# Attention and two feed-forward layers: q and k of a head loaded once, split in one tile, and copied on chip

## The reference

```python
B, H, S, D = 2, 8, 768, 64                      # 16 heads
q_bucket = sum((q @ proj > 0) * 2 ** arange(6)) # 6 hash bits for each row of q, and k_bucket of k
scores = q @ k.T / 8, or -1e9 where q_bucket != k_bucket
attn = exp(scores - max) / (sum + 1e-9)
x = (attn @ v) as 1536 tokens x 512
h = x @ w_in; g = 0 below -1, h above 1, (h + 1) ** 2 / 4 between; x = g @ w_out   # 512 -> 2048 -> 512
h = x @ w2_in; g = h - tanh(h); out = g @ w2_out
```

## Time and profile before

| | us |
|---|---|
| median of 3 runs | 813.68 (813.03 to 814.91) |
| span of the profiled execution, first to last instruction | 810.5 |
| what lies around the span, by the median | 3.2 |
| TensorE busy | 772.8 |
| attention, about | 0 to 273 |

### The profile page before, as it was taken

How to read it: one execution, slowest core, us unless ns; L and a number is a source line. 1 busy time by engine, 2 the same in 40 slices (tenths; PEclk the granted TensorE clock), 3 DMA queues, 4 the chain that set the end, 5 groups by cost and what they waited for, 6 DMA issues and landing times.

```text
span 810.5 us, 11750 instructions
## 1 busy us (share of the span) xinstructions
PE 772.8 (95%) x3712; PEld 636.0 (78%) x3712; DVE 417.4 (51%) x757; ACT 358.6 (44%) x701; POOL 326.5 (40%) x267
## 2 busy tenths in 40 slices
PE   4899999999998999999999999999999999999997
PEld 2688788788787888878887888878888888888885
DVE  2889888888898466343334455551222221231222
ACT  2788788788796343333323323331122221221221
POOL 4779789789798997000000066680000000000000
PEclk8999999999999999999999999999999999999999
DMA  6523423433221333000000022320000100010001
GB/s 202 174 89 103 147 83 103 128 102 103 78 79 53 123 114 128 1 1 0 1 1 0 0 78 104 103 79 1 0 1 1 52 0 0 0 52 0 0 0 52
DMA packets 17864, 47.25 MB, mean 58 GB/s; under 512 B 2288, under 2 KB 4464, under 8 KB 17840
## 3 DMA queue, kind: packets, MB, share of 16 engines
q1 hardware_dynamic: 17840, 46.94, 18.0%
HBM read 38.87 MB, written 3.15 MB: 52 GB/s over the span
## 4 chain that ended last, share of the span: by engine, by line
PE 71%; DVE 10%; issue 7%; POOL 4%; ACT 4%; DMA 1%; DVEq 1%; SPq 0%; ACTq 0%; POOLq 0%
PE ps L489 33%; PE ps L564 29%; PE ps L466 4%; DVE p_lo L743 3%; DVE clamped L727 2%; PE ps L423 2%; POOL probs L346 2%; POOL k_b L331 2%; PE ps L480 1%; ACT probs L610 1%; ACT p_hi L620 1%; DVE x_pair L754 1%; DVE g_raw L805 1%; DVE row_den L735 1%; DMA k_raw<-kk 1%
## 5 line engine op out<-in xcount | busy, mean ns | idle before, releaser
L489 PE MATMUL ps<-x_hi,w 128*128 (+1 forms) x768 | 255.0, 396 | 0.0
L813 DVE TENSOR_TENSOR g_lo<-g_raw,g_hi 128x512 fp32r<-128x512 f32 x96 | 71.0, 739 | 269.4 <-ACT g_hi L692 269.4
L692 ACT ACTIVATE g_hi<-g_raw 128x512 fp32r<-128x512 f32 x96 | 60.8, 633 | 296.2 <-PE ps L564 267.3
L489 PEld LDWEIGHTS ps<-x_hi,w 128*128 128x128 f32 x768 | 144.4, 188 | 33.9
L489 PE MATMUL ps<-x_lo,w 128*128 (+1 forms) x384 | 152.1, 396 | 0.0
L564 PE MATMUL ps<-g_hi,w 128*128 128x512 f32 x384 | 125.6, 391 | 3.4 <-DVE g_lo L813 3.4
L564 PE MATMUL ps<-w,g_hi 128*128 128x512 f32 x384 | 118.6, 390 | 0.0
L303 POOL TENSOR_SCALAR w<-stage 128x1024 fp32r<-128x1024 f32 x32 | 38.1, 1189 | 166.0 <-PE ps L564 164.5
L743 DVE TENSOR_TENSOR p_lo<-ps,p_hi 128x384 fp32r<-128x384 f32 x192 | 97.8, 550 | 12.6 <-ACT p_hi L620 11.4
L466 PE MATMUL ps<-ident,probs 128*128 128x128 f32 x576 | 86.3, 282 | 16.9 <-DVE p_lo L743 12.6
L346 POOL TENSOR_SCALAR probs<-probs,row_inv 128x768 f32<-128x768 f32 x96 | 86.8, 907 | 38.6 <-DVE row_inv L737 37.5
(11 more groups left out here) (48 smaller groups left out, 896.7 us busy)
## 6 DMA issues: line engine op xcount, KB each, us to landing
stage<-weights SPq DMA_DIRECT2D x32, 512.0 KB, 3.3
qk_raw<-qk SPq DMA_DIRECT2D x16, 384.0 KB, 3.5
q_raw<-qq SPq DMA_DIRECT2D x16, 384.0 KB, 3.1
k_raw<-kk SPq DMA_DIRECT2D x16, 384.0 KB, 3.9
q_a<-q_b SPq DMA_DIRECT2D x16, 192.0 KB
v_raw<-v SPq DMA_DIRECT2D x16, 192.0 KB, 2.5
out<-stage SPq DMA_DIRECT2D x12, 256.0 KB, 2.4
q_b<-bits SPq DMA_DIRECT2D x16, 54.0 KB
```

What stands on the lines that cost most here:

```text
L489: last = nc.tensor.matmul(ps[:, f % H_BANKS, :], w[:, f, wp, k * P:(k + 1) * P], xs[:, :, k, bass.ds(t * TOK, TOK)], start=(k == 0 and wp ...
L692: nc.scalar.activation(g_hi[:, slot, :], g_raw[:, slot, :], ACT.Copy).then_inc(g_hi_ready, 1)
L813: nc.vector.tensor_tensor(g_lo[:, slot, :], g_raw[:, slot, :], g_hi[:, slot, :].bitcast(F32), ALU.subtract).then_inc(g_split, 1)
```

## The change

The loads `qq` and `kk` go, `qk` (q over k, 128 rows) stays. It is scaled (rows of q by -0.125, rows of k by 1) into `qk_scaled`, rounded into `qk_hi` and subtracted into `qk_lo`, each once for q and k together, on GpSimd. Six copies on chip then bring 64 rows each to where the products read them (`copy_hi`: four, `copy_lo`: two). `qk_scaled`, `qk_hi` and `qk_lo` have one buffer, so the rounding of a head waits until the six copies of the head before have landed. The scores wait for the six parts and the two bit copies, the threshold for the bit copies of the odd head. ScalarE no longer rounds k. The hash bits of heads 0 and 1 come from products of their own (`first_products`), the first split is shared by VectorE, ScalarE and GpSimd. All pairs are written out on every engine in place of the loop. The core of the diff:

```diff
-            q_raw = sb("q_raw", [P, 2, S], F32, att)
-            k_raw = sb("k_raw", [P, 2, S], F32, att)
             qk_raw = sb("qk_raw", [P, 2, S], F32, att)
+            qk_scaled = sb("qk_scaled", [P, S], F32, att)
+            qk_hi = sb("qk_hi", [P, S], F32R, att)
+            qk_lo = sb("qk_lo", [P, S], F32R, att)
...
+            bits_odd = sb("bits_odd", [HROWS, S], F32R, att)
...
         @block.sync
         def _(sp):
             def load_qk(h, s):
-                for dst, src in ((q_raw, qq), (k_raw, kk)):
-                    sp.dma_start(dst[:, s, :], src[h, :, :]).then_inc(qk_loaded[s], 16)
+                sp.dma_start(qk_raw[:, s, :], qk[h, :, :]).then_inc(qk_loaded[s], 16)
 
             def load_v(h, s):
                 sp.dma_start(v_raw[:, s, :, :].rearrange("p t d -> p (t d)"), v[h, :, :]).then_inc(v_loaded[s], 16)
 
-            def load_pair(p):
-                for s in range(2):
-                    sp.dma_start(qk_raw[:, s, :], qk[2 * p + s, :, :]).then_inc(pair_loaded, 16)
-
-            def copy_q_hi(s):
-
-                sp.dma_start(q_a[0:D, s, :].bitcast(F32), q_b[0:D, s, :].bitcast(F32)).then_inc(rows_copied[s], 16)
-
-            def copy_bits(s):
+            def copy_hi(eng, s):
+
+                for dst, row, src in ((q_a, 0, 0), (k_a, 0, D), (k_a, D, D), (q_b, 0, 0)):
+                    eng.dma_start(dst[row:row + D, s, :].bitcast(F32), qk_hi[src:src + D, :].bitcast(F32))\
+                        .then_inc(parts_copied[s], 16)
+
+            def copy_lo(s):
+
+                for dst, row, src in ((q_a, D, 0), (k_b, 0, D)):
+                    sp.dma_start(dst[row:row + D, s, :].bitcast(F32), qk_lo[src:src + D, :].bitcast(F32))\
+                        .then_inc(parts_copied[s], 16)
+
+            def copy_bits(s, src):
 
                 for r, dst in enumerate((q_b, k_b)):
-                    row = s * HROWS + r * MROWS
                     sp.dma_start(dst[D:D + MROWS, s, :].bitcast(F32),
-                                 bits[row:row + MROWS, :].bitcast(F32)).then_inc(rows_copied[s], 16)
+                                 src[r * MROWS:(r + 1) * MROWS, :].bitcast(F32)).then_inc(bits_copied[s], 16)
+
+            def bit_rows(s):
+                return bits[s * HROWS:(s + 1) * HROWS, :]
 
             sp.dma_start(mask_s[:, :], mask_consts[:, :]).then_inc(const_loaded, 16)
-            load_pair(0)
             load_qk(0, 0)
             load_qk(1, 1)
+            sp.wait_ge(qk_hi_ready, 1)
+            copy_hi(sp, 0)
             sp.wait_ge(qk_split, 1)
-            copy_q_hi(0)
-            sp.wait_ge(bits_ready, 2)
-            copy_bits(0)
+            copy_lo(0)
+            sp.wait_ge(first_bits, 2)
+            copy_bits(0, bits[0:HROWS, :])
             load_v(0, 0)
             load_v(1, 1)
-            sp.wait_ge(bits_product, 2)
-            load_pair(1)
-            sp.wait_ge(first_k_split, 1)
+            sp.wait_ge(scale_done, 1)
+            sp.wait_ge(first_product, 4)
             load_qk(2, 0)
+            sp.wait_ge(scale_done, 2)
+            load_qk(3, 1)
 
             def pair(p):
+                first = isinstance(p, int) and p == 0
                 last = isinstance(p, int) and p == PAIRS - 1
                 before = isinstance(p, int) and p == PAIRS - 2
                 sp.wait_ge(qk_split, 2 * p + 2)
-                copy_q_hi(1)
-                copy_bits(1)
+                wait_from(sp, scores_ready, PT_TILES * p)
+                copy_hi(sp, 1)
+                copy_lo(1)
+                if first:
+                    sp.wait_ge(first_bits, 4)
+                copy_bits(1, bits_odd[:, :] if first else bit_rows(1))
                 if last:
                     return
-                load_qk(2 * p + 3, 1)
+                sp.wait_ge(qk_split, 2 * p + 3)
+                sp.wait_ge(scores_ready, PT_TILES * p + QT)
+                copy_hi(sp, 0)
+                copy_lo(0)
                 sp.wait_ge(v_split, 2 * p + 1)
                 load_v(2 * p + 2, 0)
-                if not before:
-                    sp.wait_ge(bits_product, 2 * p + 4)
-                    load_pair(p + 2)
-                sp.wait_ge(bits_ready, 2 * p + 4)
-                sp.wait_ge(qk_split, 2 * p + 3)
-                copy_q_hi(0)
-                copy_bits(0)
+                sp.wait_ge(bits_ready, 2 * p + 2)
+                copy_bits(0, bit_rows(0))
                 if not before:
                     load_qk(2 * p + 4, 0)
                 sp.wait_ge(v_split, 2 * p + 2)
                 load_v(2 * p + 3, 1)
-
-            with sp.Fori(0, PAIRS - 2) as p:
+                if not before:
+                    sp.wait_ge(scale_done, 2 * p + 4)
+                    load_qk(2 * p + 5, 1)
+
+            pair(0)
+            for p in range(1, PAIRS):
                 pair(p)
-            pair(PAIRS - 2)
-            pair(PAIRS - 1)
 
             def load_w(c, i):
...
-            def scale_q(p, s):
-
-                wait_alone(pool, qk_loaded[s], 32 * (p + 1), pool_passed)
-                pool.tensor_scalar(q_raw[:, s, :], q_raw[:, s, :], -0.125, 1.0, ALU.mult, ALU.mult)\
-                    .then_inc(q_scaled, 1)
-
-            def low_q(s):
-
-                return pool.tensor_tensor(q_a[:, s, :], q_raw[:, s, :], q_b[:, s, :].bitcast(F32), ALU.subtract)
-
-            def split_q(p, s, tiles_before):
-
-                wait_alone(pool, scores_ready, tiles_before, pool_passed)
-                wait_alone(pool, q_scaled, 2 * p + s + 1, pool_passed)
-                pool_round(q_b[:, s, :], q_raw[:, s, :]).then_inc(q_hi_ready, 1)
-                pool.wait_ge(q_hi_ready, 2 * p + s + 1)
-                low_q(s)
-
-            def split_k(p, s):
-
-                pool.wait_ge(k_hi_ready, 2 * p + s + 1)
-                pool.tensor_tensor(k_b[:, s, :], k_raw[:, s, :], k_a[:, s, :].bitcast(F32), ALU.subtract)\
+            def scale_qk(p, s):
+
+                wait_alone(pool, qk_loaded[s], 16 * (p + 1), pool_passed)
+                wait_alone(pool, qk_split, 2 * p + s, pool_passed)
+                pool.tensor_scalar(qk_scaled[:, :], qk_raw[:, s, :], qk_scale, 1.0, ALU.mult, ALU.mult)\
+                    .then_inc(scale_done, 1)
+
+            def hi_qk(p, s):
+
+                wait_alone(pool, parts_copied[1 - s], 96 * (p + s), pool_passed)
+                pool.wait_ge(scale_done, 2 * p + s + 1)
+                pool_round(qk_hi[:, :], qk_scaled[:, :]).then_inc(qk_hi_ready, 1)
+
+            def lo_qk(p, s):
+
+                pool.wait_ge(qk_hi_ready, 2 * p + s + 1)
+                pool.tensor_tensor(qk_lo[:, :], qk_scaled[:, :], qk_hi[:, :].bitcast(F32), ALU.subtract)\
                     .then_inc(qk_split, 1)
...
                         if n == 0:
-                            split_q(p, 1, PT_TILES * p)
+                            hi_qk(p, 1)
                         if n == 1:
-                            split_k(p, 1)
-                        if n == 3:
+                            lo_qk(p, 1)
+                        if n == 3 and not last:
+                            scale_qk(p + 1, 0)
+                        if n == 4 and not last:
+                            hi_qk(p + 1, 0)
+                        if n == 5 and not last:
+                            lo_qk(p + 1, 0)
+                        if n == 6:
                             split_v(p, 0)
-                        if n == 4 and not last:
-                            scale_q(p + 1, 0)
-                        if n == 6 and not last:
-                            split_q(p + 1, 0, PT_TILES * p + QT)
-                        if n == 7 and not last:
-                            split_k(p + 1, 0)
-                        if n == 10 and not last:
-                            scale_q(p + 1, 1)
-                        if n == 11:
+                        if n == 10:
                             split_v(p, 1)
+                        if n == 11 and not last:
+                            scale_qk(p + 1, 1)
...
-            scale_q(0, 0)
-            pool.wait_ge(q_hi_ready, 1)
-            low_q(0).then_inc(qk_split, 1)
-            scale_q(0, 1)
+            pool.wait_ge(const_loaded, 16)
+            scale_qk(0, 1)
             pair(0)
-            with pool.Fori(1, PAIRS - 1) as p:
+            for p in range(1, PAIRS):
                 pair(p)
-            pair(PAIRS - 1)
...
+            def first_products(s, c):
+
+                pe.wait_ge(qk_loaded[s], 16)
+                bank = ps[:, PT0 + c, 0:HALF] if s else score_bank(BITS_TURN[c])[:, 0, :]
+                nc.tensor.matmul(bank[0:2 * HROWS, :], proj_s[:, 0, :], qk_raw[:, s, c * HALF:(c + 1) * HALF],
+                                 start=True, stop=True).then_inc(first_product, 1)
+
             def bit_products(p, c):
 
-                pe.wait_ge(pair_loaded, 32 * (p + 1))
                 for s in range(2):
+                    pe.wait_ge(qk_loaded[s], 16 * (p + 1))
```

(73 more changed lines are left out.)

26 lines of the change are left out of this document (14 added, 12 removed).

## The result

The changed kernel takes 816.0 us (median of 20 runs, 814.87 to 817.71), the kernel before, run on the same chip, 813.54 us (20 runs, 808.96 to 814.91). The ratio is 1.0049, with a 95% interval of 1.0037 to 1.0062: slower by 4.0 us, where 5.9 were forecast. The profiled spans say 4.4, 814.9 against 810.5 us. The two medians are only 2.5 us apart, because the times of the kernel before fall into two groups, six of them at 809.0 to 810.1 us and fourteen at 812.5 to 814.9. That it is slower is sure; by how much is known to some 1.5 us.

What follows compares the result with a forecast made beforehand. Attention pairs were taken as bound by a chain across engines (30.91 us a period), the feed-forward part by TensorE. Start -1.65, six periods +6.7, tile 9 +0.85: +5.9 us, span 816.4, median 819.6, own range 815 to 823.5, whole range 811 to 827.

Steps and rivals of the forecast that it cites:

- Parts 1 and 2: GpSimd loses 3.7 us a pair, ScalarE two roundings; on the chain only TensorE's 0.43 us idle before the transposes goes.
- Part 3: Odd head's six copies and two bit copies, 1.29 MB at 187 GB/s, last landing at T0 + 8.35 = 118.3.
- T0: Time when the odd head's qk_lo is done and SyncE can start its copies; laid out at 109.96 us.
- point of decision: Landing of the odd head's last copies at T0 + 7.1; above it the copies bind.
- rival B: Copies in between, about 225 GB/s, landing T0 + 7.2 to 7.4, +0.2 us a pair, 813 to 814; chance 0.16.
- Part 4: TensorE's tile 6, VectorE's threshold and GpSimd's next rounding wait for the landing; threshold starts 1.24 us later.
- Part 5: Loops written out: 0.12 us a pair off for the branch; code fetching charged nothing, up to +0.5 in the range.
- Part 6: row_den's wait stays; in the last pair later copies and a vanished collision cancel, 0; tile 9's row_den adds 0.85 us.
- Rival C: Code loading or longer gaps between copies: landing slips another 0.5 to 1 us a pair, 823 to 827; chance 0.16.
- Part 7: Start of attention: with one load for head 0, copies land at 14.45, first scores 1.65 us earlier.
- Rival A: Copies overlap and only issue limits: landing T0 + 6.56 = 116.5, -0.55 us a pair, 809 us; chance 0.16.
- Rival D: Seam after attention: a shift could free the first g_raw from waiting behind GpSimd, -1.8 us; only widens the range.

Runs made afterwards that it cites:

- experiment 3: Changed kernel with the four hi copies issued once the rounding is done, only lo copies waiting for the subtraction: 808.89 us, ratio 0.9974 to the kernel before.
- experiment 1: Kernel before with only its head pairs written out on all engines instead of looped: 810.55 against 810.85 us, ratio 0.998.
- experiment 9: Kernel before, written out, with GpSimd's scaling of the next odd head and second v split moved earlier: 808.14 against 812.86 us, ratio 0.9948.
- 6: Changed kernel with hi copies issued early and GpSimd's scaling and second v split moved earlier: 804.56 us against 812.15 for the kernel before, ratio 0.991.
- experiment 8: Changed kernel with the same bytes in two 128-row and two 64-row copies, scores wrong: 809.28 us against 812.15 for the kernel before, ratio 0.9967.
- experiment 4: Changed kernel with the odd head's two bit copies issued ahead of its six parts: 824.52 us against 810.85 for the kernel before, ratio 1.0175.
- 10: As 6, with the last pair's first two weight splits at 6 and 9, not 5 and 7: 808.76 us, ratio 0.995 to the kernel before.
- 11: As 6, with only the last pair's first weight split moved, from 5 to 6: 806.52 us, ratio 0.9927 to the kernel before.
- 5: Changed kernel with GpSimd's scaling of the next odd head and second v split moved earlier: 812.38 us against 812.15 for the kernel before, ratio 1.001.
- experiment 7: Changed kernel with a seventh, unused 64-row copy for the odd head of pairs 0 to 6: 825.97 us against 812.15 for the kernel before, ratio 1.0167.

## Why the prediction was right, point by point

Its direction and its mechanism in the pair held, and the sum was 1.9 us too high (+5.9; measured +4.0 by the ratio, +4.4 by the spans). Several terms were off with opposite signs, and the step on the last pair did not hold; that the total came so close is in part luck.

- **Parts 1 and 2, work saved, and its worth.** GpSimd 29 us less, ScalarE 11; neither shortened the pair by much, as experiment 3 against 1 shows: written out both, the copies off the path, one with the saved work and one without, they have 30.60 and 30.70 us. That GpSimd's room has a worth once its steps are moved, the forecast did not see (experiment 9 against 6: 0.33 us a pair).
- **Part 3, the landing.** Forecast T0 + 8.35, measured 110.33 to 118.08, T0 + 7.75. Two of its three terms were mis-sized, in opposite directions. The packets run from 111.53 to 117.17, so they begin 1.2 us behind T0 (1.15 forecast) and take 5.6 us, not 6.9: 187 GB/s was read beside a single copy; six in a row had 234, one every 0.85 us, not 1.05. But from the last packet to the landing it took 0.9 us, not 0.3. With the right rate alone the sum would have given 7.0 to 7.1, at the point of decision of 7.1, so the short tail was made up for by the low rate. The measured landing is between the forecast and rival B. The Trainium skill, "SBUF — State Buffer", section "Door 1: The DMA port swizzle (why [64,N] ≈ [32,N])", gives 196 GB/s for 64 rows of a 1 MiB transfer and some 218 as their limit. The trace agrees in size, though its 234 is above that limit, and the measurement decides; the page's reason, half of the ports, fits experiment 8, where 128 rows move at up to 418, but no run isolates the ports. The 436 GB/s that the Trainium skill's same page gives in its summary for transfers within SBUF are approached by that run's 128-row copies only.
- **Part 4, the three waits.** All three came, with the threshold's at 118.18. Against the pair's first scores it is 0.90 us later than before (16.42 instead of 15.52 us), where 1.24 was forecast. T0 itself came 0.25 us later than laid out, against 0.6 us gained by the earlier landing. The signs named beforehand came with smaller numbers: TensorE idle 0.9 to 1.8 us before tile 6 (forecast 1.5 to 2.5), a period of 31.76 (32.0), 234 GB/s (190); GpSimd's 22 us a pair and the first scores at 14.33 fit. Experiment 3 shows the cause directly: let the copies start earlier, and the period drops by 1.16 us. GpSimd's "just ahead of the `row_den`" was right by 0.2 us, and experiment 4 shows its price.
- **Part 5, loops.** Writing out the old kernel is worth 0.2 us a pair (0.12 forecast). The slips, charged at nothing, cost some 0.4 in the mean, 0.8 in every second pair, inside the +0.5 kept for the range: the written-out kernel has +0.92 a period against before, the looped one +0.76. The Trainium skill, "Advanced Engine Details and Errata", section "ISA Cache", has 16 KB lines that hold 256 instructions; the page of the profile shows seven packets of 16 KB more. Rival C's effect exists, but in the mean it is smaller than its 0.5 to 1.
- **Part 6.** "The wait stays" held, and it is larger (0.80 for 0.59), since another instruction of GpSimd is in front: that is the 0.25 of T0. In the last pair tile 6 was 2.2 us later than before (16.56 instead of 14.40 us after the pair's first scores; 2.4 forecast), but the collision stayed: `row_den` took 2.11 us at 248.48, behind a split that was itself late. So "the two cancel" failed as a step, and so did the 0.85 for tile 9 (`row_den` took 0.17 us there). What the traces show in their place: before, TensorE has one long wait in this pair, 2.23 us at 245.42 behind `row_den`; after, it has one of 2.36 us at 245.94, for the copies, and none above 0.6 us behind `row_den`. In both the granted clock is 0.66 over 245 to 250 us. One wait took the place of the other, for a sum of +0.1 instead of +0.85; no experiment isolates this, and the forecast was close there for reasons other than its own.
- **Part 7, start.** -1.78, forecast -1.65. Pair 0 cost 0.5 us more, which was not in the sum.

In numbers: -1.78 + 0.5 + 5.5 + 0.1 = +4.4, against -1.65 + 0 + 6.7 + 0.85. The median was forecast at 819.6 and came at 816.0, and a third of that miss is not the kernel's: the 3.2 us "around the span" took the median of three runs less the span of one execution. Within one execution it is 1.9 us (816.82 and 814.9).

Rival A fails on the landing, 7.75 and not 6.56 us after T0: its copies don't overlap into a higher rate (experiment 8 shows the rate that it would have needed), and even the last issue came at T0 + 4.75 and not 4.28. Rival D fails on `g_raw`, which after still took 2.62 us.

## What to carry to other kernels

Work saved on an engine that has slack paid next to nothing here (0.1 us a pair for the 3.6 us of GpSimd's work saved in each), and the copies that replaced it started only when the last producer was done. Issue each copy as soon as its own source is ready: here that turned +4.0 us into -2.1 by the ratios. Copies on chip of 64 rows moved 234 GB/s and those of 128 rows 369 to 418, so it is worth a try to lay parts out for 128 rows; experiment 8 shows the time, with scores that are not the right ones.

Look at the smallest instructions of a profile, too. A 3-column VectorE operation that takes 0.8 us instead of 0.16 is a wait in disguise, and the cure is the order of work on the other engine, with no work taken away. Before moving such work, name what stands behind it: in experiments 10 and 11 that was the dearer wait.

## What the runs showed of the hardware

- VectorE's `row_den` (128x3) takes 0.15 to 0.17 us alone, and up to 2.35 with GpSimd in the middle of an instruction. In the 13 traces here 113 of these reads take more than 0.2 us; each began inside an instruction of GpSimd and ended 0.02 to 0.03 us behind it. The five kernels with GpSimd's steps in another order (5, 6, 9, 10, 11) moved the wait or removed it. By the Trainium skill, "SBUF — State Buffer", section "Who interferes with whom", the two share a port pair, a `tensor_scalar` like this one can take it, and whoever issues first holds it for the whole instruction; the traces agree in the times, the ports themselves they don't show.
- A late transfer can cost more than its delay. In pairs 1 to 6 of the kernel after TensorE's waits of 0.9 to 1.8 us before tile 6 left its granted clock at 1.00; in the last pair one of 2.36 did not (0.66 over 245 to 250 us); one of 1.87 (experiment 7) was followed by 0.68 over 5 us, and one of 3.8 (experiment 10) by 0.58. The length of the wait doesn't decide it alone: one of 1.83 in the same experiment 7 and one of 2.26 in experiment 9 (at 242.17) left the clock at 1.00.
- The issue of copies from SyncE's queue can stop for 1.2 us, with instruction packets in the same stretch. That the one is the other's cause was not isolated; with loops no issue in the six steady pairs took over 1 us.
- In the last pair the time depends on when a weight load lands relative to one small read: 581.4 us to the end with neither the wait nor the fall of the clock (experiment 1), 585.4 with both (kernel before); experiment 9, with the wait and without the fall, has 584.0. The kernel before itself has runs near 809.5 and near 813.5 us, the same distance apart; that the two are one thing was not tested.
